# Attention heads: where keys and queries are turned and split into two float32r parts

## The reference

```python
# attention: B=2 batches, 8 heads, S=1152 keys, head_dim 64, float32
q_pool = q.reshape(B, H, S // 2, 2, D).mean(axis=3)      # 576 queries for each batch and head
scores = (1 / sqrt(64)) * q_pool @ k^T                   # 576 x 1152
attn = softmax(scores);  attn_out = attn @ v
x = attn_out -> [1152 tokens, 512]
# then a mixture of 8 experts (top 1 of 8, 512 -> 1024 -> 512), then an MLP 512 -> 2048 -> 512
```

## Time and profile before

| what | value |
|---|---|
| time, 3 runs | 764.63, 770.3, 773.53 us; median 770.3 |
| the profiled execution | 768.31 us |
| its span, first to last instruction | 766.4 us |
| attention within the span | about 22 to 319 us |
| busy share of PE, DVE, ACT, POOL over the span | 90%, 68%, 55%, 11% |
| mean granted TensorE clock | 0.962 of full |

### The profile page before, as it was taken

The page is one execution under the profiler, slowest core; times in us unless marked ns, Lnnn a source line. Parts: engine busy times, 40 slices in busy tenths (PEclk is TensorE's granted clock), DMA queues, the critical chain, the costliest instruction groups (busy, mean ns, idle before and its releaser), DMA issues.

```text
span 766.4 us, 14706 instructions
## 1 busy us (share of the span) xinstructions
PE 687.4 (90%) x5165; PEld 608.2 (79%) x5166; DVE 523.5 (68%) x1167; ACT 417.9 (55%) x826; POOL 80.5 (11%) x80
## 2 busy tenths in 40 slices
PE   4899899999999999825999999996679999999997
PEld 3778787878788888624999899985579898989985
DVE  5666777777776776352665566666499988777884
ACT  3566466666666666302555455557366655544542
POOL 4400330303120000031000000001500000000000
PEclk9999999999999999965999999999699999999999
DMA  9964430303010100048995289111400001001001
GB/s 249 392 188 131 132 95 1 95 1 92 0 31 1 32 2 1 2 178 275 357 347 201 86 342 348 46 41 41 124 0 1 1 1 42 1 1 42 1 0 42
DMA packets 57136, 75.92 MB, mean 99 GB/s; under 512 B 22848, under 2 KB 33088, under 8 KB 56576
## 3 DMA queue, kind: packets, MB, share of 16 engines
q1 hardware_dynamic: 52736, 63.74, 24.8%
q0 software_dynamic: 2480, 8.13, 3.0%
q10 hardware_dynamic: 1872, 3.41, 1.4%
HBM read 62.42 MB, written 12.85 MB: 98 GB/s over the span
## 4 chain that ended last, share of the span: by engine, by line
PE 78%; DVE 11%; issue 4%; DMA 2%; ACT 2%; POOL 1%; DVEq 0%; SPq 0%; POOLq 0%; ACTq 0%
PE score_banks L854 13%; PE score_banks L817 13%; PE score_banks L831 9%; PE turn L655 9%; PE pvT L638 8%; PE score_banks L871 4%; PE turn L871 4%; PE pvT L871 4%; PE score_banks L614 4%; PE score_banks L615 4%; PE turn L596 2%; DVE nmax_part L1058 2%; DVE nmax_part L1051 1%; DVE qT L1070 1%; DVE qT L1069 1%
## 5 line engine op out<-in xcount | busy, mean ns | idle before, releaser
L655 PE MATMUL turn<-ident,prob 128*128 128x128 f32 x648 | 110.3, 280 | 17.5 <-DVE x_tok L1092 11.9
L1051 DVE TENSOR_REDUCE nmax_part<-score_banks 128x1 f32<-128x768 f32 x72 | 68.9, 957 | 61.3 <-PE score_banks L615 49.5
L655 PEld LDWEIGHTS turn<-ident,prob 128*128 128x128 f32 x648 | 78.9, 142 | 36.8 <-DVE probT L1103 19.9
L817 PEld LDWEIGHTS score_banks<-xsT,w_slot 128*128 128x128 f32 x832 | 96.9, 196 | 5.4 <-issue 4.6
L817 PE MATMUL score_banks<-xsT,w_slot 128*128 x832 | 97.8, 280 | 3.1 <-issue 1.6
L900 ACT ACTIVATE prob<-score_banks,nmax 128x1152 f32<-128x1152 f32 x72 | 87.6, 1217 | 9.4 <-DVE nmax L1061 9.3
L638 PE MATMUL pvT<-probT,v_sb 128*64 128x128 f32 (+1 forms) x1440 | 87.2, 267 | 0.0
L1195 DVE TENSOR_TENSOR w_lo<-w_slot,w_hi 128x512 fp32r<-128x512 f32 x104 | 71.8, 692 | 19.1 <-ACT w_hi L965 19.0
L614 PE MATMUL score_banks<-kT,qT 128*128 128x384 f32 x192 | 82.4, 429 | 1.5 <-DVE qT L1070 1.5
L638 PEld LDWEIGHTS pvT<-probT,v_sb 128*64 128x64 f32 x1440 | 70.6, 137 | 12.0 <-issue 11.9
L907 ACT ACTIVATE probT<-turn 128x384 f32<-128x384 f32 x72 | 35.3, 491 | 78.0 <-PE turn L655 78.0
(11 more groups left out here) (158 smaller groups left out, 1382.8 us busy)
## 6 DMA issues: line engine op xcount, KB each, us to landing
w_slot<-moe_w SPq DMA_DIRECT2D x16, 2048.0 KB, 13.8
raw_k<-k SPq DMA_DIRECT2D x16, 288.0 KB, 3.9
v_sb<-v SPq DMA_DIRECT2D x16, 288.0 KB, 4.1
slots_dram<-zeros SPq DMA_DIRECT2D x72, 64.0 KB, 1.6
raw_q<-q SPq DMA_DIRECT2D x16, 256.0 KB, 3.6
w_in_sb<-moe_w_in SPq DMA_DIRECT2D x1, 4096.0 KB, 13.2
w_out_sb<-moe_w_out SPq DMA_DIRECT2D x1, 4096.0 KB, 14.9
stage<-slots_dram ACTq DMA_DIRECT2D x13, 256.0 KB, 2.7
```

Of the source, the lines that this page charges most:

```text
L655: last = pe.transpose(bank[:, j * P:(j + 1) * P], prob[:, s % 2, c * KC + j * P:c * KC + (j + 1) * P], ident[:, :])
L817: last = pe.matmul(h1_bank[f % 4][:, 0:P], w1_e[:, d, f * P:(f + 1) * P], xsT[:, d, bass.ds((t % XS_RING) * P, P)], start=(d == 0), stop=( ...
L1051: dve.tensor_reduce(nmax_part[:, s, 0:1], scores[s % 2][:, lo:lo + 2, 0:KC], AX.XY, ALU.max, negate=True).then_inc(max_part, 1)
```

## The change

Keys and queries are no longer split before they are turned.

- **Turning.** Head h's keys (`raw_k`) and summed queries (`q_pair`) are laid out with both batches side by side: 64 columns of batch 0, 64 of batch 1. One 128x128 turn handles a tile of both batches. A head takes 9 turns of keys and 5 of queries, in five groups (PREPS = 5): queries at i = 0 (three turns) and i = 1 (two turns), keys at i = 2, 3 and 4. Steps 5 to 8 have no preparatory turn. The result has head dims of batch 0 in partitions 0 to 63 and of batch 1 in 64 to 127.
- **Splitting.** ACT copies the turned groups to `q_turned` (640 columns) and `k_turned` (3 x 384 columns). POOL splits behind that: queries high and low in one piece each, keys high and low for each third. POOL still does the sum of the queries, for head n+1, ahead of the split of head n.
- **Stacking.** SP moves the parts with 12 SBUF-to-SBUF DMAs a head (`restack`): 8 for the queries, 4 for the keys, each 64 partitions by 512 to 1152 columns. PE waits for them (`stacked[0]`, before the first scores of the next head at i = 7, and `stacked[1]` at its tile 4). `swap_parts` is gone.
- **First head.** PE turns unsplit keys and queries into five banks, ACT writes the high parts and DVE the low ones straight from PSUM, 9 units each. The main loop begins after the first scores of tile 1.
- **SP's order.** Head loads are issued earlier, expert 0 after the first `restack`, expert 1 after the second. The 72 DMAs of zeros become 4 (2304 runs of 512 bytes each), one behind each of four later heads.

The core of the diff:

```diff
+            def restack(h):
+                par = h % 2
+                sp.wait_ge(q_split, h)
+                for b in range(B):
+                    src = slice(b * DH, (b + 1) * DH)
+                    at, n = (0, Q0 * P) if b == 0 else (Q0 * P, FT * P)
+                    for var in range(2):
+                        hi, lo = slice(var * DH, (var + 1) * DH), slice((1 - var) * DH, (2 - var) * DH)
+                        sp.dma_start(qT[hi, par, var, at:at + n].bitcast(F32), q_hi[src, 0:n].bitcast(F32)
+                                     ).then_inc(stacked[b], 16)
+                        sp.dma_start(qT[lo, par, var, at:at + n].bitcast(F32), q_lo[src, 0:n].bitcast(F32)
+                                     ).then_inc(stacked[b], 16)
+                sp.wait_ge(k_split, NC * h)
+                for b in range(B):
+                    src, cols = slice(b * DH, (b + 1) * DH), slice(b * S, (b + 1) * S)
+                    sp.dma_start(kT[0:DH, par, cols].bitcast(F32), k_hi[src, :].bitcast(F32)).then_inc(stacked[b], 16)
+                    sp.dma_start(kT[DH:2 * DH, par, cols].bitcast(F32), k_lo[src, :].bitcast(F32)).then_inc(stacked[b], 16)
...
+            load_kq(1)
             load_v(0, 0)
+            sp.wait_ge(first_turned, NC + 2)
+            load_kq(2)
+            load_v(1, 1)
+            restack(1)
...
-            sp.wait_ge(zeros_ready, 1)
-            for d in range(DT):
-                for t in range(DRAM_TILES):
-                    sp.dma_start(slots_dram[t * P:(t + 1) * P, d * P:(d + 1) * P], zeros[:, :]
-                                 ).then_inc(xs_zeroed, 16)
...
+            for h in range(1, NH - 1):
+                if h + 2 < NH:
+                    sp.wait_ge(prep_turned, PREPS * h)
+                    load_kq(h + 2)
+                sp.wait_ge(pv_done, GH * h)
+                load_v(h + 1, (h + 1) % 2)
+                restack(h + 1)
+                if h == 1:
+                    load_expert(1, 1)
+                elif h - 2 < ZERO_PARTS:
+                    sp.wait_ge(zeros_ready, 1)
+                    sp.dma_start(flat_slots[:, (h - 2) * zeros_per:(h - 1) * zeros_per, :],
+                                 zeros[:, :].unsqueeze(1).broadcast_to([P, zeros_per, P])).then_inc(xs_zeroed, 16)
...
+            def split(n, first):
+                pool.wait_ge(prep_copied, PREPS * (n - 1) + 2)
...
+                pool.tensor_copy(q_hi[:, :], q_turned[:, :]).then_inc(hi_done, 1)
+                pool.wait_ge(hi_done, (NC + 1) * (n - 1) + 1)
+                pool.tensor_tensor(q_lo[:, :], q_turned[:, :], q_hi[:, :].bitcast(F32), ALU.subtract).then_inc(q_split, 1)
+                for c in range(NC):
+                    cols = slice(c * KC, (c + 1) * KC)
+                    pool.wait_ge(prep_copied, PREPS * (n - 1) + 3 + c)
+                    pool.tensor_copy(k_hi[:, cols], k_turned[:, cols]).then_inc(hi_done, 1)
+                    pool.wait_ge(hi_done, (NC + 1) * (n - 1) + 2 + c)
+                    pool.tensor_tensor(k_lo[:, cols], k_turned[:, cols], k_hi[:, cols].bitcast(F32), ALU.subtract
+                                       ).then_inc(k_split, 1)
...
+            for n in range(1, NH):
+                if n + 1 < NH:
+                    pool_q_sum((n + 1) % 2, (n + 1) // 2 + (n + 1) % 2)
+                split(n, n == 1)
...
-                        if i2 == 0:
-                            pe.wait_ge(q_swapped, NQ * h2 + 1)
-                        elif i2 == 2:
-                            pe.wait_ge(prep_copied, TPH * h2 + TPH)
-                            pe.wait_ge(q_swapped, NQ * h2 + NQ)
+                        if first and s + 2 < TPH:
+                            if i2 == FT:
+                                pe.wait_ge(first_ready, len(first_units))
+                        elif i2 == 0:
+                            pe.wait_ge(stacked[0], 16 * RESTACK * h2)
+                        elif i2 == FT:
+                            pe.wait_ge(stacked[1], 16 * RESTACK * h2)
...
-                    if s % TPH - 1 in q_chunks and not (final and s >= TPH):
-                        swap_parts(HB * it + s // TPH + 1, (s // TPH + 1) % 2, s % TPH - 1)
```

More of the change, by code:

```diff
@@ L273, in build @@
         v_landed = [sem(f"v_landed{n}") for n in range(2)]
[L274 to L278, removed]
+        q_summed = sem("q_summed")
+        hi_done = sem("hi_done")
+        q_split = sem("q_split")
+        k_split = sem("k_split")
+        stacked = [sem(f"stacked{b}") for b in range(B)]
         prep_turned = sem("prep_turned")
@@ L304, in build, with q_sum, first_rows @@
         block = ctx.enter_context(nc.Block())
[L308 to L312, removed]
+        tile_at = list(range(FT)) + [B * FT] + list(range(FT, B * FT))
+        slot_at = [tile_at.index(i) for i in range(TPH)]
+        first_bank = [turn[0], turn[1], score_banks[:, 0, :], pvT, score_banks[:, 1, :]]
+        FIRST_Q, FIRST_TAIL = NC, NC + 1
+        first_units = [("k", 0, 0), ("k", 0, 1), ("k", 0, 2), ("q", 0, FIRST_Q), ("k", 1, 2), ("k", 1, 0),
+                       ("q", 0, FIRST_TAIL), ("k", 1, 1), ("q", 1, FIRST_Q)]
+        FIRST_Q_READY, FIRST_BANK0_FREE, FIRST_BANK1_FREE, FIRST_TURN_FREE = 4, 5, 7, 8
+        def q_sum(eng, par, part):
+            if part == 0:
+                raw = raw_q[:, par, 0:B * FT, :].rearrange("p (b i) d -> p b i d", b=B)
+                dst = q_pair[:, par, 0:FT, :, :].rearrange("p i b d -> p b i d")
+            else:
+                raw = raw_q[:, par, B * FT:, :].broadcast_to([P, B, 2 * DH])
+                dst = q_pair[:, par, FT, :, :]
+            lo, hi = slice(0, DH), slice(DH, 2 * DH)
+            if part == 0:
+                return eng.tensor_tensor(dst, raw[:, :, :, lo], raw[:, :, :, hi], ALU.add)
+            return eng.tensor_tensor(dst, raw[:, :, lo], raw[:, :, hi], ALU.add)
+        def first_rows(unit):
+            kind, b, c = unit
+            here, there = slice(b * DH, (b + 1) * DH), slice((1 - b) * DH, (2 - b) * DH)
+            if kind == "k":
+                at, n = b * S + c * KC, KC
+            elif c == FIRST_TAIL:
+                at, n = FT * P, P
+            else:
+                at, n = (0, FT * P) if b == 0 else (Q0 * P, FT * P)
+            return here, there, slice(at, at + n), first_bank[c][here, 0:n]
         logit_parts = [(0, 0, 0, TC), (DH, 1, TC, TC), (0, 2, 2 * TC, TC - 1), (DH, 0, 3 * TC - 1, 1)]
@@ L421, in split, with preps_before @@
[L421 to L437, removed]
+        def preps_before(h, i, last_head):
+            return PREPS * h + (i if last_head else min(i, PREPS))
@@ L547, in _, with pool_q_sum @@
                                base=0, pattern=[[-1, P]], channel_multiplier=1).then_inc(ident_ready, 1)
-            split(pool, 0, 1, True)
+            def pool_q_sum(par, landings):
+                pool.wait_ge(q_landed[par], 16 * 2 * B * landings)
+                q_sum(pool, par, 0)
+                q_sum(pool, par, 1).then_inc(q_summed, 1)
+            def split(n, first):
+                pool.wait_ge(prep_copied, PREPS * (n - 1) + 2)
+                if not first:
+                    for b in range(B):
+                        pool.wait_ge(stacked[b], 16 * RESTACK * (n - 1))
+                pool.tensor_copy(q_hi[:, :], q_turned[:, :]).then_inc(hi_done, 1)
[8 more added lines that the diff above has]
+                                       ).then_inc(k_split, 1)
+            pool_q_sum(1, 1)
             pool.memset(zeros[:, :], 0.0).then_inc(zeros_ready, 1)
@@ L648, in pv_begin @@
                     pe.wait_ge(v_landed[k // GH], 16 * B * (it + 1))
[L649 removed]
+                if isinstance(it, int) and it == 0 and k == 0:
+                    pe.wait_ge(first_ready, len(first_units))
+                else:
                     pe.wait_ge(o_copied, GB * it + k)
```

235 lines of the change are left out of this document (133 added, 102 removed).

## The result

The changed kernel takes 743.92 us (median, 739.67 to 744.6) against 770.36 for the kernel before (764.63 to 773.53). The ratio is 0.965, 95% interval 0.960 to 0.971: 26 us faster. The prediction was 750, range 738 to 764. The profiled execution took 739.67 us, span 738.0, against 768.31 and 766.4.

What follows compares the result with a forecast made beforehand. PE was taken to bound attention, losing some 2 us a head to DVE's order. Heads 11.9, zeros 3.9 and start 4 sum to 19.8 us off 768.3: 748.5, plus 2.0 for the median gives 750, range 738 to 764.

Steps and rivals of the forecast that it cites:

- likeliest case: Attention heads: some collisions of POOL with `nmax`, chance 0.47; this case alone 744 to 756 us.
- PE's work of 33.02 us a head: Steady heads: PE's work after the change, summed over nine intervals, 33.02 us against 36.61 before.
- Turns and swaps: Steady heads: 13 fewer PE turns save 1.47 us a head, waits behind DVE's swap casts 2.12.
- chains that do not shrink: Steps without preparatory turns: other engines' chains must still fit, adding 0.3 us a head, 33.3 in all.
- bad case: Steady heads: POOL's split always ahead of `nmax`, costing 2.6 us a head, 1.4 of it at the queries' step i = 1.
- no collision: Rival for steady heads: `nmax` always first, gains of 7 x 3.3 + 3.9 + 4 = 31, 739 us; chance 0.18.
- Restack: Stacking DMAs before `stacked[0]` at i = 7: hidden beside PE's work, cost nothing, margin 1.4 us.
- restack late: Rival: stacking DMAs late by 1 to 2 us a head, losing 7 to 14 us, 757 to 764 us; chance 0.11.
- Zeros: Second head: 72 zero DMAs delay head 3's loads and cause the 8.73 us interval; four DMAs win back 3.9 us.
- case of the lower bound: Zeros term: gain only 2 us if loads behind 4 MB of an expert's weights come late once.
- Start: Before the main loop: first turn at about 16.5 us wins 5, DVE's wait gives back 1; 4 us credited, from 1 to 6.
- POOL's term: Steady heads: collisions of POOL's split with `nmax` cost 1.3 us a head, the sum of queries 0.3.

Runs made afterwards that it cites:

- Experiments 2: Changed kernel with two idle DVE casts of 64 x 384 put back where the swaps stood (i = 4, 5 and 7): 753.66 us, ratio 0.981.
- experiment 3: Changed kernel with 13 PE turns of the identity a head put back, nothing copied out of them: 748.49 us, ratio 0.977.
- experiment 4: Changed kernel with both the idle DVE casts and the 13 identity turns a head put back: 756.24 us, ratio 0.981.
- experiment 6: Changed kernel without POOL's casts and subtractions for heads 1 to 7: 779.68 us, total not comparable because routing changes; heads 3 and 4 last 33.82 and 33.64 us.
- experiment 7: Changed kernel with POOL's split in smaller pieces (queries 512 and 128 columns, keys 256 and 128): 751.76 us, ratio 0.978.
- Experiment 5: Changed kernel with the keys' stacking DMAs of batch 1 issued ahead of those of batch 0: 754.83 us, ratio 0.983.
- experiment 1: Kernel before the change, with only its 72 DMAs of zeros issued as 4: ratio 0.997.
- Experiment 8: Changed kernel with head loads ahead of expert weights: 741.01 us; also with DVE's last first-head unit moved into the first step: 740.78; changed kernel beside them 743.78.

## Why the prediction was right, point by point

The measured 743.92 us lies inside the range, 6 us below the forecast of 750 and just outside the 744 to 756 of the likeliest case. The mechanism held: PE sets the pace, it needs fewer turns and waits less for DVE. The case that I called likeliest did not happen, though. I forecast collisions with POOL in some steps; in the steady heads there was none, which is the rival that I gave 0.18. That the number still fits owes something to the width of the range.

**Bound and method.** PE's order of instructions sets a step, and the three long intervals were mostly DVE's doing. Experiments 2 and 3 show both, each alone; a small part at i = 8 was a wait for ACT's copy (experiment 4). PE's work of 33.02 us a head is what the kernel approaches: the real head is 33.7, and the 0.7 above it are the waits of the next paragraph.

**Turns and swaps.** I had 1.47 and 2.12 us a head, less 0.3 for chains that do not shrink. The total is 2.8, not 3.3, so the 0.3 should have been 0.7. Of it 0.2 to 0.4 stand at i = 8 (3.45 to 3.61 against the 3.20 of PE's work), the rest as 0.1 each at i = 2, 5 and 7. At i = 5, 7 and 8 PE's weight load waits for ACT's copy of the last third (the changed kernel, timeline, i = 7 and 8):

```profile
151.43 0.31 PEld L730 LDWEIGHTS turn<-ident,prob 128*128 128x128 f32 x3 [0.20 <-ACT probT L988]
...
155.15 0.31 PEld L730 LDWEIGHTS turn<-ident,prob 128*128 128x128 f32 x3 [0.30 <-ACT probT L988]
```

The chain exponential, copy, next turn is longer than PE's own work there once three turns are gone. I had named this chain but priced it from DVE's side. The 0.1 at i = 2 goes when the one turn at i = 1 is put back (experiment 3); which engine PE waits for there the trace does not name.

**POOL.** The term that was mis-sized most: 1.6 us a head (1.3 for the split, 0.3 for the sum of queries), 11 us in all; measured nothing in a steady head and 0.8 to 1.4 us in heads 1 and 2 together. For the split experiment 6 shows it. For the sum only the trace speaks: it stretched `nmax` to 0.48 and 0.47 us in two heads, and the interval around it kept its 3.87. The mechanism was right, and experiment 7 shows it, but my price for the bad case was too high: 2.6 us a head with POOL always first, of which 1.4 at the queries' step. There 1.3 to 1.4 a head and 1.0 at that step were measured, with pieces that are shorter (1.27 us instead of 1.55). What whole pieces would cost was not run. That the two start within 0.1 us of each other was right too. But I took half of the bad case as the likeliest. Every steady head repeats the same timing, so the answer is the same in all its steps: it is all or nothing, and a mean of two ends is a value that hardly occurs. Which of the two it would be could not be read from 2.39 against 2.4: that `nmax` came first is luck as far as the forecast goes. The rival "no collision" with 739 us was nearer than the forecast's sum. The Trainium skill, "SBUF — State Buffer", section "Who interferes with whom", says that a VectorE instruction with two SBUF inputs contends with a GpSimd instruction that reads SBUF, and that the one that issues first keeps the port to its end while the other waits. The trace agrees for `nmax`, which took 0.16 us when it was 0.01 us ahead and 1.19 when it was 0.09 behind.

**Restack.** Hidden, as forecast. The margin was 0.6 us, not 1.4, because I took 4.5 us from the ready low part to the landing and it was 5.5 (142.05 to 147.6). The estimate from the same page's section on the DMA port swizzle had led to about 1.3 us more than my row; what was missing is 1.0, so that estimate was nearer here than the row of a load that fills 128 partitions. That the ports are the reason is not shown: two more DMAs and a part of the zeros are in flight behind these two, and no run moves the same bytes without them. Experiment 5 shows what the rival "restack late" costs: 1.3 us too late, 1.5 us a head.

**Zeros.** Cause right, gain of 3.9 us right for that interval. My claim that four DMAs don't hold SP long holds for the changed kernel, not for experiment 1, where they stand behind the weights. The case of the lower bound (loads behind 4 MB late once) happened, in head 2, at a price of 0.5 to 1.2 us.

**Start.** 4 us credited, 2.9 and 3.8 measured in the two profiles, which differ in the granted clock (0.76 and 0.81 against 1.00 between 20 and 28 us). The loop's first turn came at 17.57 us (I had about 16.5), 4.3 us earlier than before, and the wait for DVE in the first step was 2.0 us, not 1. Experiment 8 confirms that DVE's last unit was most of it.

**Sum.** 19.8 us forecast, 25.1 measured in attention: the heads' ordinary part gave 18.3 instead of 11.9, the long interval 3.9 as forecast, the start 2.9 instead of 4. Of the 6.4 us too little in the heads, POOL's term is 10 the one way and the chains that do not shrink are 3 the other way.

## What to carry to other kernels

Cut a steady loop into intervals by one recurring instruction and add up the bound engine's own work in each: what is above the sum is a wait for another engine, here mostly the order of DVE's queue, and it can be worth as much as the work that a change takes away. Where two engines meet at a shared port within a tenth of a microsecond in a repeating pattern, forecast two cases with a chance each, not their mean, and read after the run which one it is. A transfer that is hidden should be shifted once on purpose; the margin is part of the result.

## What the runs showed of the hardware

- A DVE tensor_tensor of one column took 0.16 us, 1.19 us or 0.73 us, by whether it started 0.01 us before or 0.09 and 0.02 us after a GpSimd tensor_tensor; a reduction from PSUM beside POOL kept its 0.55 us. A DVE cast of 64x384 took 1.14 us instead of 0.42 beside a GpSimd cast (the kernel before, 81.82 us).
- A stacking DMA from SBUF to SBUF of 64 partitions by 4608 bytes landed 4.4 to 5.0 us after its issue, one of 64 by 2560 or 2048 bytes after 2.6 to 3.2. Loads of the keys, now issued right behind them and, in three heads, behind the zeros, went from 3.9 us to 5.4.
- 1152 KB of zeros in 2304 runs of 512 bytes took 8.5 us in one DMA.
- Behind the PE wait of 2.86 us the granted clock was 0.94 of full from 84 to 88 us and 0.63 from 88 to 92, which comes to half for about 3.4 us; in the changed kernel it is 1.00 in every stretch of 4 us from 28 us to the end of attention.
